# An mLSTM with two MLPs on one core: two heads over each other in the rows of queries, keys and state

## The reference

```python
for t in range(S):
    m_new = max(f_gate[t] + m, i_gate[t])
    f_stab, i_stab = exp(f_gate[t] + m - m_new), exp(i_gate[t] - m_new)
    C = f_stab * C + i_stab * outer(v[t], k[t])      # 40 x 40 per head
    n = f_stab * n + i_stab * k[t]
    y[t] = sigmoid(o_gate[t]) * (C @ q[t]) / max(abs(n @ q[t]), 1)
```

```python
h = relu(x @ w_in); u, v = h[:512], h[512:]
x = (u * (w_spatial @ layernorm(v) + b_spatial)) @ w_out
xk, xr = mix(mu_k, x, x_prev), mix(mu_r, x, x_prev)
y = sigmoid(xr @ w_r) * (relu(xk @ w_k) ** 2 @ w_v)
```

## Time and profile before

| | |
|---|---|
| median of 3 runs | 337.61 us (336.91 to 337.61) |
| profiled execution, its own time | 336.92 us |
| its span, first to last instruction | 335.2 us |
| TensorE busy | 318.3 us (95%) |
| VectorE busy | 211.6 us (63%) |
| ScalarE busy | 141.2 us (42%) |
| GpSimd busy | 69.5 us (21%) |
| mean granted clock of TensorE | 0.994 |
| moved by DMA | 20.94 MB |

### The profile page before, as it was taken

The page is one execution under the profiler, slowest core; times in us unless marked ns, Lnnn a source line. Parts: engine busy times, 40 slices in busy tenths (PEclk is TensorE's granted clock), DMA queues, the critical chain, the costliest instruction groups (busy, mean ns, idle before and its releaser), DMA issues.

```text
span 335.2 us, 5769 instructions
## 1 busy us (share of the span) xinstructions
PE 318.3 (95%) x2112; PEld 303.2 (90%) x2112; DVE 211.6 (63%) x448; ACT 141.2 (42%) x272; POOL 69.5 (21%) x94
## 2 busy tenths in 40 slices
PE   8879899999999999787999999999799999999996
PEld 3879789999999989677999999999699999999996
DVE  7889788566366555754553398978679636856011
ACT  5955673133332332352311345447685146336100
POOL 8713322012201200150211120115031013013000
PEclk9999999999999999999999999999799999999999
DMA  6972223312253115400003202040000100010011
GB/s 206 282 223 77 50 60 80 74 39 63 69 133 95 32 42 187 127 2 0 1 2 116 73 0 59 3 145 12 2 0 2 59 2 2 20 41 0 22 40 58
DMA packets 9815, 20.94 MB, mean 62 GB/s; under 512 B 1788, under 2 KB 5388, under 8 KB 9308
## 3 DMA queue, kind: packets, MB, share of 16 engines
q1 hardware_dynamic: 9788, 20.58, 21.2%
HBM read 18.53 MB, written 1.97 MB: 61 GB/s over the span
## 4 chain that ended last, share of the span: by engine, by line
PE 75%; DVE 15%; issue 4%; ACT 4%; POOL 1%; DVEq 0%; ACTq 0%; POOLq 0%
PE ps_v L1061 17%; PE ps_s L1061 10%; PE ps_e L1061 7%; PE ps_in L1061 6%; PE ps_out L1061 6%; PE ps_t L1061 6%; PE ps_in L1140 5%; PE ps_out L1150 4%; PE ps_s L1131 4%; PE ps_z L1061 4%; PE ps_z L1159 2%; DVE kr L1033 1%; PE ps_e L1107 1%; PE ps_e L1112 1%; DVE pt L792 1%
## 5 line engine op out<-in xcount | busy, mean ns | idle before, releaser
L526 POOL TENSOR_TENSOR kkl<-kr,kkh 128x384 fp32r<-128x384 f32 x16 | 17.6, 1097 | 73.2 <-ACT kkh L682 73.2
L1033 DVE TENSOR_TENSOR kr<-kr 128x384 f32<-128x384 f32 x32 | 20.4, 641 | 14.4 <-ACT kr L725 14.3
L1131 PEld LDWEIGHTS ps_s<-qkt 128*128 128x128 f32 x192 | 24.7, 191 | 1.5
L1131 PE MATMUL ps_s<-qkt 128*128 128x128 f32 x192 | 25.6, 276 | 0.0
L1140 PEld LDWEIGHTS ps_in<-tok,pt 128*128 128x128 f32 x192 | 24.1, 191 | 1.3
L1140 PE MATMUL ps_in<-tok,pt 128*128 128x42 f32 x192 | 24.7, 279 | 0.0
L561 ACT ACTIVATE et<-ps_e 128x512 f32<-128x512 f32 x24 | 14.3, 595 | 24.6 <-PE ps_e L1112 20.9
L698 ACT ACTIVATE gh<-ut 128x384 fp32r<-128x384 f32 x16 | 8.4, 525 | 33.4 <-DVE ut L998 33.3
L1061 PE MATMUL ps_v<-win,xth 128*128 128x512 f32 x60 | 20.8, 411 | 1.3 <-DVE xtl L867 1.3
L521 POOL TENSOR_TENSOR gl<-ut,gh 128x384 fp32r<-128x384 f32 x8 | 9.5, 1183 | 58.5 <-ACT gh L698 58.5
L1061 PE MATMUL ps_v<-xth,win 128*128 128x384 f32 x65 | 19.1, 359 | 2.5 <-ACT vr L567 1.4
(11 more groups left out here) (293 smaller groups left out, 918.5 us busy)
## 6 DMA issues: line engine op xcount, KB each, us to landing
tok<-in_vk SPq DMA_DIRECT2D x12, 328.0 KB, 4.7
qkt<-in_qk SPq DMA_DIRECT2D x12, 320.0 KB
sp_raw<-in_w_sp SPq DMA_DIRECT2D x6, 384.0 KB, 5.4
osig<-in_og SPq DMA_DIRECT2D x2, 960.0 KB, 10.6
out_y<-ob SPq DMA_DIRECT2D x12, 160.0 KB, 1.7
wv_raw<-in_w_v SPq DMA_DIRECT2D x2, 640.0 KB, 5.0
win_raw<-in_w_in SPq DMA_DIRECT2D x4, 256.0 KB, 7.9
wk_raw<-in_w_k SPq DMA_DIRECT2D x2, 512.0 KB, 4.3
```

The costliest lines, as they stand in the source:

```text
L526: gp.tensor_tensor(kkl[a % 2][:, b, :], kr[n % 4][:, :], bits(kkh[a % 2][:, b, :]), ALU.subtract).then_inc(sems["kk_lo_pool"], 1)
L1033: ve.tensor_tensor(kr[n % 4][:, :], kr[n % 4][:, :], kr[n % 4][:, :], ALU.mult).then_inc(sems["kk_done"], 1)
L1131: last = te.matmul(ps_s[j][:, h * CH:(h + 1) * CH], qkt[:, u % NS, 1, cols], qkt[:, u % NS, 0, cols], start=True, stop=True)
```

## The change

Heads h and h+4 are laid over each other: head h in rows 0 to 39, head h+4 in rows 64 to 103.

- The queries take four blocks of 128 tokens instead of eight, each with both heads of a pair. The keys keep eight blocks; the rows of the pair's other head hold zeros in them. A place in `qkt` has 1536 columns instead of 2048.
- The state `zt` is [128 rows, 4 pairs, 2 heads, 42], with zeros in the other head's rows, so one product with 84 moving columns gives the carried part of two heads. `carry` has 4 products instead of 8; its output is written to the two heads' places in `p_out`.
- `kw` holds a pair of heads over 128 columns (40, 24 zeros, 40, 24 zeros), of which 104 are the weights; `state` has 4 products with 84 moving columns. The off-diagonal quarters of the result are not read.
- `state_add` is two instructions, one for each half of the rows. `decay_state` runs over 104 rows.
- Queries and keys come by two DMAs per chunk, one for each half of the rows; the scores wait for 32 instead of 16.
- The fills of `qkt` follow its new size; `kw` gets one on GpSimd ahead of that of `zt`.

```diff
+G = H // 2
+QK = (G + H) * CH
...
-    qkt = at("qkt", [KR, NS, 2, H * CH], STK)
+    qkt = at("qkt", [KR, NS, QK], STK)
+    queries = [qkt[:, n, 0:G * CH].rearrange("p (g t) -> p g t", g=G) for n in range(NS)]
+    keys = [qkt[:, n, G * CH:QK].rearrange("p (h t) -> p h t", h=H) for n in range(NS)]
...
-    kw = tail("kw", [128, H, D])
+    kw = tail("kw", [128, G, 128])
-    zt = [tail(f"zt{n}", [KR, H, DV]) for n in range(2)]
-    zdec = tail("zdec", [D, H, DV])
+    zt = [tail(f"zt{n}", [KR, G, 2, DV]) for n in range(2)]
+    zdec = tail("zdec", [ER, G, 2, DV])
...
-                    sp.wait_ge(sems[f"pad{u}"], 2)
-                sp.dma_start(qkt[0:D, u % NS, :, :], qk[u]).then_inc(sems[f"qk_in{u % NS}"], 16)
+                    sp.wait_ge(sems[f"pad{u}"], 2 if u == 0 else 1)
+
+                for r in range(2):
+                    parts = qkt[64 * r:64 * r + D, u % NS, :].rearrange("p (x t) -> p x t", x=3)
+                    sp.dma_start(parts[:, 0:r + 2:r + 1, :],
+                                 qk[u][:, :, r * HH * CH:(r + 1) * HH * CH]).then_inc(sems[f"qk_in{u % NS}"], 16)
...
-            gp.memset(qkt[:, 0, 1, :], 0.0).then_inc(sems["pad0"], 1)
+            gp.memset(qkt[:, 0, 0:QK // 2], 0.0).then_inc(sems["pad0"], 1)
...
-            gp.memset(qkt[:, 2, 0, :], 0.0).then_inc(sems["pad2"], 1)
-            gp.memset(qkt[:, 2, 1, :], 0.0).then_inc(sems["pad2"], 1)
+            gp.memset(qkt[:, 2, :], 0.0).then_inc(sems["pad2"], 1)
             gp.memset(bits(mrow[:, 1, :, :, :]), 0.0).then_inc(sems["rows_one_zero"], 1)
+            gp.memset(kw[:, :, :], 0.0).then_inc(sems["kw_zero"], 1)
...
-                w = gwt[:, c, 64 + GW * b:64 + GW * b + H].unsqueeze(2).broadcast_to([128, H, D])
-                gp.tensor_tensor(kw[:, :, :], kt[u % 2], w, ALU.mult).then_inc(sems["kw_done"], 1)
+                w = gwt[:, c, 64 + GW * b:64 + GW * b + H].rearrange("p (r g) -> p g r", r=2)
+                gp.tensor_tensor(kw[:, :, :].rearrange("p g (r d) -> p g r d", r=2)[:, :, :, 0:D],
+                                 kt[u % 2].rearrange("p (r g) d -> p g r d", r=2),
+                                 w.unsqueeze(3).broadcast_to([128, G, 2, D]), ALU.mult).then_inc(sems["kw_done"], 1)
...
-                d = dec[0:D, c, GW * b:GW * b + H].unsqueeze(2).broadcast_to([D, H, DV])
-                gp.tensor_tensor(zdec[:, :, :], zt[(u - 1) % 2][0:D, :, :], d, ALU.mult).then_inc(sems["z_decayed"], 1)
+                d = dec[0:ER, c, GW * b:GW * b + H].rearrange("p (r g) -> p g r", r=2)
+                gp.tensor_tensor(zdec[:, :, :, :], zt[(u - 1) % 2][0:ER, :, :, :],
+                                 d.unsqueeze(3).broadcast_to([ER, G, 2, DV]), ALU.mult).then_inc(sems["z_decayed"], 1)
...
-            for n in range(2):
-                sc.activation(qkt[:, 1, n, :].rearrange("p (x t) -> p x t", x=2),
-                              vr[:, :].unsqueeze(1).broadcast_to([KR, 2, HF]), ACT.Copy).then_inc(sems["pad1"], 1)
+            sc.activation(qkt[:, 1, :].rearrange("p (x t) -> p x t", x=3),
+                          vr[:, :].unsqueeze(1).broadcast_to([KR, 3, HF]), ACT.Copy).then_inc(sems["pad1"], 1)
...
-                    ve.tensor_copy(z, p_z[0:D, :, :]).then_inc(sems["z_added"], 1)
                 else:
                     dve.wait_ge(sems["z_decayed"], decay_no(u) + 1)
-                    ve.tensor_tensor(z, p_z[0:D, :, :], zdec[:, :, :], ALU.add).then_inc(sems["z_added"], 1)
+                for r in range(2):
+                    rows = slice(64 * r, 64 * r + D)
+                    z, new = zt[u % 2][rows, :, r, :], p_z[rows, :, r, :]
+                    if chunk(u) == 0:
+                        last = ve.tensor_copy(z, new)
+                    else:
+                        last = ve.tensor_tensor(z, new, zdec[rows, :, r, :], ALU.add)
+                last.then_inc(sems["z_added"], 1)
...
-            ve.memset(qkt[:, 0, 0, :], 0.0).then_inc(sems["pad0"], 1)
+            ve.memset(qkt[:, 0, QK // 2:QK], 0.0).then_inc(sems["pad0"], 1)
...
-                    cols = slice((HH * j + h) * CH, (HH * j + h + 1) * CH)
-                    last = te.matmul(ps_s[j][:, h * CH:(h + 1) * CH], qkt[:, u % NS, 1, cols],
-                                     qkt[:, u % NS, 0, cols], start=True, stop=True)
+                    last = te.matmul(ps_s[j][:, h * CH:(h + 1) * CH], keys[u % NS][:, HH * j + h, :],
+                                     queries[u % NS][:, h, :], start=True, stop=True)
...
-                for h in range(H):
-                    last = te.matmul(p_out[:, h, :], qkt[:, u % NS, 0, h * CH:(h + 1) * CH],
-                                     zt[(u - 1) % 2][:, h, :], start=True, stop=True)
+                for g in range(G):
+                    last = te.matmul(p_out.rearrange("p (r g) d -> p r g d", r=2)[:, :, g, :],
+                                     queries[u % NS][:, g, :], zt[(u - 1) % 2][:, g, :, :], start=True, stop=True)
...
-                for h in range(H):
-                    last = te.matmul(p_z[0:D, h, :], kw[:, h, :], vt[u % 2][:, h, :], start=True, stop=True)
+                for g in range(G):
+                    last = te.matmul(p_z[0:ER, g, :, :], kw[:, g, 0:ER],
+                                     vt[u % 2].rearrange("p (r g) d -> p g r d", r=2)[:, g, :, :],
+                                     start=True, stop=True)
```

More of the change, by code:

```diff
@@ L144 @@
 gate_m gate_next gates_in group_mm gwt_done head_rows_done ident_done ident_zero later_done later_zero ones_done k_relu
-kk_done kk_hi_done kk_lo_dve kk_lo_pool kw_done mix_biased mix_gated mrow_in
+kk_done kk_hi_done kk_lo_dve kk_lo_pool kw_done kw_zero mix_biased mix_gated mrow_in
 mu_done mu_in nm_hi_done nm_zero nm_lo_done num_done o_in0 o_in1 osig_done out_done0 out_done1 out_ready
@@ L296, in by_head @@
             return bank[:, 0:H * DV].rearrange("p (h d) -> p h d", d=DV)
-        p_in, p_out, p_z = by_head(ps_in), by_head(ps_out), by_head(ps_z)
+        p_in, p_out = by_head(ps_in), by_head(ps_out)
+        p_z = ps_z[:, 0:H * DV].rearrange("p (g r d) -> p g r d", g=G, r=2)
         p_factors = ps_t[:, 3 * CH:3 * CH + ER]
@@ L456, in _ @@
             head_rows(0, 1)
-            gp.memset(qkt[:, 2, 0, :], 0.0).then_inc(sems["pad2"], 1)
-            gp.memset(qkt[:, 2, 1, :], 0.0).then_inc(sems["pad2"], 1)
+            gp.memset(qkt[:, 2, :], 0.0).then_inc(sems["pad2"], 1)
             gp.memset(bits(mrow[:, 1, :, :, :]), 0.0).then_inc(sems["rows_one_zero"], 1)
-            gp.memset(zt[0][:, :, :], 0.0)
-            gp.memset(zt[1][:, :, :], 0.0).then_inc(sems["zt_zero"], 1)
+            gp.memset(kw[:, :, :], 0.0).then_inc(sems["kw_zero"], 1)
+            gp.memset(zt[0][:, :, :, :], 0.0)
+            gp.memset(zt[1][:, :, :, :], 0.0).then_inc(sems["zt_zero"], 1)
             pool.wait_ge(sems["zt_zero"], 1)
@@ L803, in state_add @@
                 n = state_no(u)
-                z = zt[u % 2][0:D, :, :]
                 dve.wait_ge(sems["state_mm"], n + 1)
@@ L1125, in scores @@
             def scores(u, j):
-                pe.wait_ge(sems[f"qk_in{u % NS}"], 16 * (u // NS + 1))
+                pe.wait_ge(sems[f"qk_in{u % NS}"], 32 * (u // NS + 1))
                 if u > 0 or j > 0:
```

## The result

The changed kernel takes 332.85 us (median of 6 runs, 330.76 to 334.84), the kernel before, run beside it, 337.55 (336.82 to 338.91): a ratio of 0.986, 95% interval 0.9818 to 0.9902. It is faster, as forecast, but by 4.7 us and not 7.2, and the time lies outside the range. The profiled execution took 331.42 (span 329.7).

The account below looks back on a forecast made before the run. VectorE was taken to bound the kernel up to about 51 us, TensorE from there to the attention's end near 136. Carried -6.27, state -1.14, addition +0.4, fills -0.2 gave -7.2: 336.9 to 329.7 us, range 327.6 to 332.2.

Parts of the forecast that it names:

- Carried and state products: TensorE, 51 to 136 us: seven carried chunks save 6.27 us, six states save 1.14.
- no gain: Rival: a product costs by its moving columns, 84 twice as much as 42; 337.1 us, chance 0.03.
- the slower rival: Wide carried products, writing two PSUM pieces, lose their overlap; up to 348.5 us, chance 0.04.
- the loss at the ends: TensorE, scores ahead of and values behind a state's narrow block: 0.19 us lost per state, expected to go.
- dearer states: Rival: eight state loads at full pace, end losses kept, +2.0 us; 331.7, chance 0.14.
- State addition: VectorE: one instruction becomes two, 0.1 us more each, four on its chain up to 51 us: +0.4.
- The fills: Smaller first-slot fill of qkt at the front of the chain: 0 to 0.23 us saved, 0.2 taken.
- Loads: Queries and keys by two DMAs, SP issuing one more: cost nothing, +0.5 us as the other end.
- GpSimd's products: kw and zdec in another order: cost nothing; a slower kw could lengthen VectorE's normalisation by 0 to 0.5 us.
- The start of the profiled execution: VectorE's chain up to 51 us: addition +0.4 and fills -0.2, so 0.2 us longer.
- The median: Whole kernel: profiled execution forecast at 329.7 us, a median perhaps some tenths above.
- The one rival on the clock: The clock's fall from 236 us, 1.7 us lost, doesn't come once work has moved: 328.0, chance 0.10.

Follow-up runs that it names:

- a_busy: Changed kernel plus unread products in six idle stretches of TensorE: 329.18 us, ratio 0.9737 to the kernel before.
- a_state8: Changed kernel with the state written by eight narrow products, each into its own head's rows and columns: 333.02 us, ratio 0.9826 to the kernel before.
- a_rows4k: Changed kernel with queries and keys laid out so each half load is whole rows of 4 KB: 332.73 us, ratio 0.9835 to the kernel before.
- b_two_loads: Kernel before with each chunk's queries and keys loaded by two DMAs instead of one: 338.95 us, ratio 1.0024 to the kernel before.
- a_one_add: Changed kernel with one state addition over rows 0 to 103, carried part not the reference's: 330.08 us, ratio 0.9788 to the kernel before.
- a_both: Changed kernel with whole 4 KB rows and one state addition, carried part not the reference's: 332.13 us, ratio 0.9792 to the kernel before.
- c_best_busy: Changed kernel with 4 KB rows, narrow state and one addition in the first four chunks, plus unread products in idle stretches: 328.10 us, ratio 0.9708.
- a_again: Changed kernel repeated without an edit: 332.42 us, ratio 0.9819 to the kernel before.
- b_busy: Kernel before plus unread products in six idle stretches of TensorE: 335.78 us, ratio 0.9927 to the kernel before.
- c_best: Changed kernel with 4 KB rows and, in the first four chunks, narrow state over a cleared bank and one addition: 330.60 us, ratio 0.9806.
- a_twice: Changed kernel with the carried products of chunks 1 to 3 issued twice: 332.18 us, ratio 0.9817 to the kernel before.
- a_warm: Changed kernel plus 20 products that no one reads, in slots 1 and 3: 332.43 us, ratio 0.9843 to the kernel before.

## Why the prediction was right in direction and wrong in size

**Carried and state products: right.** 7.4 us forecast, 7.4 found between the spread and the end of the attention, in after and in a_busy (51.82 to 129.31, 77.5). The pace of 0.112 held for 84 columns in two pieces of PSUM, so neither "no gain" nor the slower rival came about. The Trainium skill (SBUF — State Buffer, Door 1: The DMA port swizzle) has such pieces slow a matmul significantly; this output, 42 columns and again 42, didn't. The state's block cost what was forecast, and a_state8 brought the loss at the ends back with narrow weights: "dearer states" fell. The Trainium skill (TensorEngine Tiling, Key Properties: changing the mode drains the TensorE) agrees with that.

**State addition: the mis-sized term.** +0.1 each was taken, 0.15 was the upper end, 0.28 was measured. The two didn't overlap at all, and each half took 0.33 where the line through two sizes gave 0.32; what was compared with 490 ns, the row's duration, should have been the 0.41 after which the next instruction starts. Four of them are 1.1 us instead of 0.4. The fills gave 0.26, forecast 0.2. In a_busy, without falls, the start is 51.82 - 50.96 = 0.86 longer, about 1.1 - 0.26.

**Loads: nothing, as forecast, though their issue was dearer than it took it for.** "SP issues one more" was counted as one issue; in fact each of the two took 0.81 us instead of 0.28 to 0.41. Taking that away (a_rows4k) or bringing it into the kernel before (b_two_loads) didn't move the time.

**GpSimd's products: put at nothing, and that holds in some executions only.** The prediction let a slower kw lengthen VectorE's normalisation by up to 0.5. What came was a late kw: it waited for the tokens of chunk 2, and then ran beside VectorE's outputs. In after this reads:

```profile
29.98 0.74 POOL L480 TENSOR_TENSOR kw<-tok,gwt 128x320 f32<-128x320 f32 x1 [2.43 <-DMA tok<-in_vk]
30.03 0.72 DVE L858 TENSOR_SCALAR den<-den 128x8 f32<-128x8 f32 x1
```

The second row takes 0.17 elsewhere, so 0.55 was lost. In a_one_add it was 0.23, in a_both and c_best_busy, both with whole rows, about 0.4; in a_again, a_rows4k and a_busy nothing. So it isn't shown to come from the dearer issue; why the tokens land late in one execution and not in another is open.

**The start of the profiled execution.** The forecast had it 0.2 longer, and it was 1.74: 0.86 as in a_busy, 0.55 from kw, and 0.32 up to L844 in chunk 0 (18.91; 18.59 in a_busy), of which 0.22 is a wait for the values. So 1.5 of the 1.7 us by which this execution, 331.42, missed 329.7 are the start.

**The median: the step that failed most.** "A median may be some tenths above 329.7." It took the profiled execution of before, 336.92 with one fall of the clock, as its usual one. The runs of before beside all sets say otherwise: 335.43 to 335.47 at clock 1.000, 336.86 to 337.02 at 0.994 to 0.995, mostly 338.4 to 338.6 at 0.990, 338.8 to 340.0 at 0.984 and 0.985. By these steps a fall costs 1.5 us on average, and the usual execution has two or three. The one rival on the clock let the fall go away; none let more come. In the first comparison before stood 337.55 - 335.45 = 2.1 above its time at full clock, after 332.85 - 329.18 = 3.7 above a_busy (whose unread products may cost some 0.3 themselves: b_busy is that much above 335.45). The forecast had 1.5 of falls in it. So 329.7, plus 0.6 for the gain of 6.6 in place of 7.2, plus 2.2 for the falls, is 332.5 of 332.85. This is a split and not a check: the part of the falls is itself a difference of medians, taken on two chips. The ends of the prediction's own terms, all at once, are 326.4 and 333.1 and not its 327.4 and 332.5: 332.85 lay within them, and outside the range that was cut narrower.

**What the falls come from.** Shown: idle of TensorE. Filling six idle stretches took all of them away, in all three kernels where it was done (b_busy, a_busy, c_best_busy). The Trainium skill (TensorE: Matmul & The Clock Gate, Loop structure matters more than you think) says the same of a loop that waits between its matmuls. That the changed kernel has more of them is likely: the mean clock of 12 runs of after and a_again is 0.978, that of the 45 runs of before beside the three sets 0.986. The single values overlap, but of the 42 runs with the change and without added products (after, a_again, a_rows4k, a_one_add, a_both, a_state8, c_best) none was above 0.990, and of those 45 eleven were at 0.994 or more. Not shown is why. a_twice, which gave TensorE its old work back in three chunks, still had its falls, and b_two_loads, which has the two loads alone, had a fall at 16 to 28 and a slightly lower clock. Open too is why the 20 products of a_warm narrowed the times without lowering the median. They fill early stretches only, where VectorE mostly sets the pace; the later falls (232 in its profile, 148 and 232 in a_again's) stayed. That fits, but wasn't tested by itself.

## What to carry to other kernels

Cost a float32 product by what paces it in the rows (here the width of its weights, not its moving columns), and a split of a VectorE instruction by when the next one can start, not by its duration. Before the sum is set against a time, look at the granted clock of several runs: an execution with one fall is no base for a kernel that usually has two or three. Where TensorE waits for other engines in short stretches, a few products that no one reads may be worth more than an edit: 3.1 us of 338.9 here, and times that then lie within 0.3 us, in which small edits can be seen at all.

## What the runs showed of the hardware

- A DMA from SP whose 40 rows lie in two pieces of 2 KB took 0.81 us to issue (median of 24), one with whole rows of 4 KB 0.33, one with whole rows of 8 KB 0.28 to 0.41. In the kernel before with two loads it was the same 0.81, so it is the pieces and not the target.
- A fall of the clock at 36 to 44 cost nothing in one kernel (c_best), one at 16 to 28 cost about 2 us in another (b_two_loads), and one at 40 to 52 put a spread off by 3.4 us (a_twice): what it costs depends on how long it lasts and on whether TensorE or VectorE ends last there.
- Sixteen narrow records take 0.75 us one after the other into the same rows and 0.63 when neighbours alternate between rows 0 to 39 and 64 to 103. That the alternation is the reason wasn't tested.
